# VectorE instead of TensorE turns q and k in an attention with hashed masks and two feed-forward layers

## The chip, the cores and the metric

The kernel runs on one core of one Trainium2 chip. The metric is the time of one execution on the device in microseconds (us); lower is better. The engines of a core work side by side and wait for each other through semaphores only: TensorE (PE, with its weight loads as PEld), VectorE (DVE), ScalarE (ACT), GpSimd (POOL), and SyncE (SP), which here issues nearly all DMA transfers.

## What is computed

Everything is in 32-bit floats. There are 2 batches of 8 heads, 768 positions and 64 columns a head; the output of attention, 1536 x 512, goes through two feed-forward layers.

```python
scale = 1.0 / np.sqrt(D)
q_bits = (np.einsum('bhsd,dk->bhsk', q, proj) > 0).astype(np.int64)
k_bits = (np.einsum('bhsd,dk->bhsk', k, proj) > 0).astype(np.int64)
mask = q_bucket[:, :, :, None] == k_bucket[:, :, None, :]   # buckets: the 6 bits as a number
scores = scale * np.matmul(q, k.transpose(0, 1, 3, 2))
scores = np.where(mask, scores, -1000000000.0)
scores = scores - np.max(scores, axis=-1, keepdims=True)
attn = np.exp(scores)
attn = attn / (np.sum(attn, axis=-1, keepdims=True) + 1e-09)
x = np.matmul(attn, v)
h = np.maximum(np.maximum(x @ w1, x @ w2), x @ w3) @ w_out
g = h @ w_in
out = (g * (1.0 / (1.0 + np.exp(-1.702 * g)))) @ w_out2
```

## The kernel before

The program is written out engine by engine: each engine has its own list of instructions in a fixed order, and every dependence is a wait on a semaphore. An engine never goes past an instruction that waits.

**Heads and tiles.** The 16 heads are taken in 8 pairs. A head's scores are made 128 rows of queries by 768 keys at a time (a score tile); 96 tiles in all. The main loop runs over groups n = 4 to 32 of three tiles each, 3n, 3n+1 and 3n+2, called A, B and C below; four groups make a pair of heads, p = n // 4, st = n % 4. Groups 0 to 3 are written out one by one.

**One group on TensorE.** In order: scores of A (L1522, four matmuls into the PSUM banks psS), three half tiles of probabilities turned with the identity (`turn_probs`, L1530, nine transposes into the ring of three banks psR), scores of B, three more half tiles, scores of C behind them in the next turn of the loop. Between B and C stand twelve matmuls with the values (`times_values`, L1544, into psO) and, depending on st, one of three things: at st 0 and 1 `turn_qk` (L1470), which turns q and k of one head of the next pair, six transposes of 128x128; at st 2 `project` (L1500), which multiplies the turned q and k of both heads with proj; at st 3 nothing. In this text a group's halves are turned as "D": the order on the engine is C, D, A, D, B, values, then the next C.

**The chain of one tile.** VectorE takes the maximum over the scores in PSUM (`row_max`, L1128), ScalarE the exponential with its sum (`exp_tile`, L803), VectorE the guarded sums and their reciprocals (`invert_sums`: lone L1136, lone_sums L1137, guarded L1142, inv L1145), GpSimd the normalization in place (`norm`, L577), TensorE turns it, and ScalarE (L812) or VectorE (L1152) copies the halves out of the ring. Two score banks (psS) mean that the scores of tile i wait for the exponential of tile i − 2. A and B are inverted together, so their lone and lone_sums work on two columns, those of C on one. At even n VectorE also makes x_lo (L1158) between the inversion of A and B and the maximum of C.

**One head's q and k before the scores.** SP loads them (`load_qk`, L436) into w_raw, as rows of positions with q and k side by side: 128 partitions, runs of 64 columns (256 bytes). TensorE turns them into two ring banks. ScalarE copies the banks out (`copy_qk`, L796), with a scale that is −1/8 on the 64 partitions of q and 1 on those of k. GpSimd splits the result into a high part (qk_hi, L560) and the rest (qk_lo, L573), which follow the two norms of its group. SP places the parts into stacks (`place_hi`, `place_lo`, `place_marks`), from which the scores are made one pair later. Buffers for loaded, turned and split heads are there twice, so head m uses those of head m − 2.

GpSimd has more work in some groups: from n = 16 on, at st 2 and 3, three sums of x each (L626), and in the last four groups the first block of weights. Behind attention come the feed-forward layers on TensorE, with their weights split by GpSimd and ScalarE.

Of the kernel before, what the change touches and what calls it, by code (L numbers as in the profile page):

```python
# [5 lines left out]
def lsh_attention_ffn(nc, q, k, v, proj, w1, w2, w3, w_out, w_in2, w_out2, out):  # L6
# [3 lines left out]
    ts = bass.ts  # L10
# [74 lines left out]
    k_r = k.rearrange("b h (p t) d -> (b h) p t d", p=P)  # L85
    v_r = v.rearrange("b h (p t) d -> (b h) p t d", p=P)
    w_up = [w.rearrange("(c p) f -> p c f", p=P) for w in (w1, w2, w3)]
    w_out_r = w_out.rearrange("(c p) d -> p c d", p=P)
# [6 lines left out]
    for n_ in range(GROUPS + 1):  # L95
        p_, st = n_ // 4, n_ % 4
        halves = [("probs", i, j) for i in range(3 * n_ - 3, 3 * n_) for j in range(2)] if n_ > 0 else []
        if n_ == 2:

            ring_order += halves[:2] + [("bits", 1)] + halves[2:]  # L100
            continue
        ring_order += halves[:3]
        if st < 2 and p_ + 1 < PAIRS:
            ring_order += [("turn", 2 * p_ + 2 + st, j) for j in range(2)]
        if st == 2 and p_ + 1 < PAIRS:
            ring_order += [("bits", p_ + 1)]
        ring_order += halves[3:]
# [3 lines left out]
    with ctx:  # L111
# [55 lines left out]
        sum_of_w = sb("sum_of_w", [P, SLOT], F32)  # L167
        qk_raw = [w_raw[:, ts(a, S)].rearrange("p (t s d) -> p t s d", s=2, d=D) for a in range(2)]
        qk_t = [w_raw[:, ts(2 + a, S)] for a in range(2)]
        qk_hi = [w_hi[:, ts(a, S)] for a in range(2)]  # L170
# [88 lines left out]
        dve_stacked = sem("dve_stacked")  # L259
        pool_stacked = sem("pool_stacked")  # L260
        qk_hi_made = sem("qk_hi_made")
        qk_lo_made = sem("qk_lo_made")
# [86 lines left out]


        def hi_stacked(m):
            return hi_placed[m % 2], 64 * (m // 2)
# [75 lines left out]
        def _(sync):  # L428
            def load_qk(m):
                if m >= 4:  # L430
                    sync.wait_ge(*filled(("turn", m - 2, 1)))
                elif m >= 2:
                    sync.wait_ge(first_turned, 2 * (m - 1))
                for which, src in enumerate((q_r, k_r)):
                    if m >= 2 or which == 0:
                        sync.dma_start(qk_raw[m % 2][:, :, which, :], src[m, :, :, :]).then_inc(qk_loaded[m % 2], 16)  # L436
# [28 lines left out]
            def load_block(k):  # L465
                if k == 0:
                    sync.wait_ge(*filled(("turn", HEADS - 1, 1)))
                elif k < 3:
                    sync.wait_ge(*filled(("bits", PAIRS - 1)))
                    sync.wait_ge(qk_lo_made, HEADS - 2)  # L470
                else:
                    sync.wait_ge(w_split, part_use[k - 2, "a11"])
                fp, c = k // 3, k % 3
                sync.dma_start(w_raw[:, ts(k % 3, BLOCK_COLS)].rearrange("p (c f) -> p c f", c=KC),
                               w_up[c][:, :, ts(fp, SLOT)]).then_inc(w_loaded[k % 3], 16)
# [75 lines left out]
        def _(pool):  # L551
# [10 lines left out]
            def make_qk_hi(m):  # L562
                for j in range(2):
                    pool.wait_ge(*emptied(("turn", m, j)))
                if m >= 4:
                    pool.wait_ge(*hi_stacked(m - 2))
                copy(qk_hi[m % 2], qk_t[m % 2]).then_inc(qk_hi_made, 1)
# [220 lines left out]
        def _(act):  # L788
            def copy_qk(m, j):
                act.wait_ge(*filled(("turn", m, j)))  # L790
                if m in (2, 3):
                    act.wait_ge(dve_stacked, m + 1)
                    act.wait_ge(pool_stacked, (2, 6)[m - 2])
                if m >= 4:
                    act.wait_ge(qk_lo_made, m - 3)
                act.activation(half(qk_t[m % 2], j), bank(("turn", m, j))[:, 0:HALF], ACT.Copy,  # L796
                               scale=qk_scale[:, 0:1]).then_inc(bank_emptied(("turn", m, j)), 1)

            def exp_tile(i):
# [81 lines left out]
            for n in range(4, GROUPS + 1):  # L881
# [9 lines left out]
                if st < 2 and p + 1 < PAIRS:  # L891
                    for j in range(2):
                        copy_qk(2 * p + 2 + st, j)
                copy_turned(3 * n - 2, 1)
# [214 lines left out]
        def _(dve):  # L1109
# [11 lines left out]
            def make_first_bits(a):  # L1121
                dve.wait_ge(*filled(("bits", 0, a)))
                dve.tensor_scalar(first_marked[a], bank(("bits", 0, a))[:, 0:HALF], marks[:, 2:3], marks[:, 3:4], ALU.is_gt,
                                  ALU.mult).then_inc(bank_emptied(("bits", 0, a)), 1)

            def row_max(i):
                dve.wait_ge(scores_ready, i + 1)
# [96 lines left out]
            row_max(11)  # L1224
            copy_turned(8, 1)
            for n in range(4, GROUPS + 1):
                p, st = n // 4, n % 4
# [4 lines left out]
                if n < GROUPS:  # L1232
                    row_max(3 * n + 1)
                    invert_sums(3 * n, 2)
                    if st == 2 and p + 1 < PAIRS:
                        make_bits(p + 1)
# [221 lines left out]
        def _(pe):  # L1458
# [33 lines left out]
            def project(p):  # L1492
                for a in range(2):
                    for j in range(2):
                        pe.wait_ge(*emptied(("turn", 2 * p + a, j)))
                o = ring_bank(("bits", p))
# [103 lines left out]
            for n in range(4, GROUPS + 1):  # L1600
# [9 lines left out]
                for c in range(TH * part, TH * part + TH):  # L1610
                    times_values(u, c)
                if st < 2 and p + 1 < PAIRS:
                    turn_qk(2 * p + 2 + st)
                if st == 2 and p + 1 < PAIRS:
# [177 lines left out]
```

## Time and profile before

| | us |
|---|---|
| median of 3 runs | 672.41 (672.07 to 672.5) |
| span of the profiled execution, first to last instruction | 670.8 |
| TensorE busy | 663.7 (99%) |
| VectorE busy | 495.9 (74%) |
| ScalarE busy | 346.6 (52%) |
| GpSimd busy | 474.2 (71%) |
| clock granted to TensorE, mean | 1.000 of full speed |

The span is from the profile; of the profiled execution the profile gives no time other than this span, and the median of the separate runs is 1.6 us above it. Busy times are sums over the instructions of an engine, and those of matmuls are modelled, so that 99% doesn't mean that TensorE couldn't go faster; what it waits for is read from the chain and the timeline. Attention takes the first 230 us or so.

### The profile page before, as it was taken

How to read it: one execution, taken by the hardware profiler on the slowest of the kernel's cores; microseconds unless marked ns; L12 is line 12 of the kernel's file. 1: busy time of each engine (PE TensorE's matmuls, PEld its weight loads, DVE VectorE, ACT ScalarE, POOL GpSimd, SP SyncE). 2: the span in 40 equal slices, each digit the busy share in tenths (PEclk: the TensorE clock that was granted, in tenths of full speed). 3: DMA queues.
4: the chain of work that ended last, by engine and by line, in shares of the span. 5: the costliest groups of instructions: out<-in, count | busy, mean ns of one | idle time of the engine just before them, and what ended most of it. 6: DMA issues, size and time to landing. Idle time of an engine off the chain costs nothing.

```text
span 670.8 us, 11966 instructions
## 1 busy us (share of the span) xinstructions
PE 663.7 (99%) x3892; PEld 576.8 (86%) x3892; DVE 495.9 (74%) x976; ACT 346.6 (52%) x761; POOL 474.2 (71%) x538
## 2 busy tenths in 40 slices
PE   8999999999999999999999999999999999999998
PEld 6776777777777699999999999988898988989896
DVE  6878878788788799869778963678877666555554
ACT  6887777877777630011103453555545554454433
POOL 6774756788876899968870528799987776777710
PEclk9999999999999999999999999999999999999999
DMA  6673836638352111111110201212232124212102
GB/s 159 152 161 102 192 88 155 151 88 187 91 132 75 34 32 32 32 32 33 32 40 25 95 1 33 79 48 80 79 93 64 64 78 143 64 64 65 45 18 94
DMA packets 58492, 54.17 MB, mean 81 GB/s; under 512 B 28640, under 2 KB 47488, under 8 KB 58432
## 3 DMA queue, kind: packets, MB, share of 16 engines
q1 hardware_dynamic: 56784, 53.02, 29.2%
q8 instruction: 32, 0.52, 0.3%
q10 hardware_dynamic: 1648, 0.39, 0.3%
q14 instruction: 28, 0.23, 0.1%
HBM read 32.51 MB, written 3.15 MB: 53 GB/s over the span
## 4 chain that ended last, share of the span: by engine, by line
PE 88%; POOL 6%; issue 2%; ACT 1%; DVE 1%; DMA 1%; DVEq 0%; ACTq 0%; POOLq 0%
PE psO L1544 10%; PE psS L1522 10%; PE psR L1530 9%; PE psR L1628 7%; PE psR L1627 7%; PE psR L1629 7%; PE psS L1627 6%; PE psS L1628 6%; PE psS L1629 6%; PE psS L1730 4%; PE psS L1729 4%; PE psS L1728 4%; POOL w_lo L736 3%; PE psR L1470 1%; POOL w_raw L727 1%
## 5 line engine op out<-in xcount | busy, mean ns | idle before, releaser
L577 POOL TENSOR_SCALAR probs<-probs,lone,inv 128x768 f32<-128x768 f32 x96 | 93.9, 985 | 58.6 <-DVE inv L1145 58.5
L736 POOL TENSOR_TENSOR w_lo<-w_raw,w_hi 128x256 fp32r<-128x256 f32 x96 | 79.2, 838 | 44.6 <-ACT w_hi L982 43.9
L1128 DVE TENSOR_REDUCE neg_max<-psS 128x1 f32<-128x768 f32 x96 | 91.2, 950 | 12.9 <-PE psS L1522 8.7
L803 ACT ACTIVATE probs<-psS,neg_max 128x768 f32<-128x768 f32 x96 | 86.5, 901 | 15.7 <-DVE neg_max L1128 15.6
L560 POOL TENSOR_SCALAR w_hi<-w_raw 128x256 fp32r<-128x256 f32 (+1 forms) x79 | 49.0, 624 | 50.2 <-PE psS L1629 28.9
L812 ACT ACTIVATE probs_t<-psR 128x384 f32<-128x384 f32 x131 | 60.7, 491 | 31.2 <-PE psR L1530 30.7
L1530 PE MATMUL psR<-ident,probs 128*128 128x128 f32 x576 | 74.6, 273 | 0.4 <-POOL probs L577 0.2
L1530 PEld LDWEIGHTS psR<-ident,probs 128*128 128x128 f32 x576 | 66.5, 140 | 5.5 <-POOL probs L577 2.1
L1544 PE MATMUL psO<-probs_t,v_raw 128*64 128x384 f32 x384 | 68.8, 494 | 0.0
L1379 DVE TENSOR_TENSOR v_raw<-psR,early 128x384 f32<-128x384 f32 x64 | 35.3, 552 | 32.4 <-PE psR L1629 32.2
L1384 DVE TENSOR_TENSOR v_raw<-v_raw,bits 128x384 f32<-128x384 f32 x64 | 53.7, 841 | 6.7 <-ACT bits L1005 4.3
L1628 PE MATMUL psR<-x_lo,w_hi 128*128 128x384 f32 x160 | 53.8, 337 | 0.0
L1629 PE MATMUL psR<-x_hi,w_lo 128*128 128x384 f32 x160 | 53.6, 335 | 0.0
L1627 PE MATMUL psR<-x_hi,w_hi 128*128 128x384 f32 x160 | 53.4, 334 | 0.0
L1005 ACT ACTIVATE bits<-v_raw 128x384 f32<-128x384 f32 x64 | 33.5, 524 | 35.9 <-DVE v_raw L1379 35.7
L1544 PEld LDWEIGHTS psO<-probs_t,v_raw 128*64 128x64 f32 x384 | 24.8, 136 | 30.8 <-issue 30.5
L741 POOL TENSOR_TENSOR w_parts<-w_raw,w_parts 128x512 fp32r<-128x512 f32 x32 | 42.1, 1339 | 8.4 <-ACT w_parts L990 8.4
L597 POOL TENSOR_TENSOR w_lo<-w_raw,w_hi 128x256 fp32r<-128x256 f32 x52 | 46.0, 890 | 0.3
L982 ACT ACTIVATE w_hi<-w_raw 128x256 fp32r<-128x256 f32 x87 | 31.9, 406 | 27.0 <-POOL w_raw L727 24.4
L1379 DVE TENSOR_TENSOR early<-psR,early 128x384 f32<-128x384 f32 x48 | 26.5, 552 | 25.8 <-PE psR L1629 25.6
L1302 DVE TENSOR_TENSOR probs_t<-probs_t,v_raw 128x384 f32<-128x384 f32 x48 | 35.0, 748 | 0.0
L1152 DVE COPY probs_t<-psR 128x384 f32<-128x384 f32 x61 | 33.6, 551 | 0.7
(275 smaller groups left out, 1881.5 us busy)
## 6 DMA issues: line engine op xcount, KB each, us to landing
w_raw<-in_moe_w_in SPq DMA_DIRECT2D x16, 512.0 KB, 3.4
w_raw<-in_moe_w_out SPq DMA_DIRECT2D x32, 256.0 KB, 2.7
w_raw<-in_moe_w SPq DMA_DIRECT2D x9, 512.0 KB, 3.8
h_lo<-w_hi SPq DMA_DIRECT2D x22, 192.0 KB, 3.3
h_hi<-w_hi SPq DMA_DIRECT2D x18, 192.0 KB, 3.4
w_raw<-in_q SPq DMA_DIRECT2D x16, 192.0 KB, 3.6
v_raw<-in_v SPq DMA_DIRECT2D x16, 192.0 KB, 2.5
stacks<-w_hi SPq DMA_DIRECT2D x16, 192.0 KB, 3.3
```

The costliest lines, as they stand in the source:

```text
L577: pool.tensor_scalar(probs[i % PROBS][:, :], probs[i % PROBS][:, :], lone[:, i % 6:i % 6 + 1], inv[:, i % 6:i % 6 + 1], ALU.add, ALU.mult) ...
L736: pool.tensor_tensor(in2_slot(w_lo, n, which), in2_raw(n, PARTS2[which]), f32(in2_slot(w_hi, n, which)), ALU.subtract).then_inc(in2_split, 1)
L803: act.activation(probs[i % PROBS][:, :].rearrange("p (a b) -> p a b", a=2), psS[i % 2][:, :, 0:HALF], ACT.Exp, bias=neg_max[:, i % 6:i % 6 ...
L812: act.activation(probs_t[u % 2][:, s // TH, ts(j, TH), ts(s % TH, P)], bank(("probs", i, j))[:, 0:HALF].rearrange("p (c q) -> p c q", c=TH ...
L1128: dve.tensor_reduce(neg_max[:, i % 6:i % 6 + 1], psS[i % 2][:, :, 0:HALF], AX.XY, ALU.min).then_inc(max_ready, 1)
L1379: dve.tensor_tensor(o, psU[(7 * n + product) % 2], other, ALU.add).then_inc(mix_added, 1)
L1522: mm = pe.matmul(psS[i % 2][:, j, 0:HALF], stack(n, qs)[0:rows, ts(t, P)], half(stack(n, ks)[0:rows, :], j), start=which == 0, stop=which ...
L1530: mm = pe.transpose(o[:, ts(c, P)], probs[i % PROBS][:, ts(j * TH + c, P)], ident[:, :])
L1544: mm = pe.matmul(psO[a * D:(a + 1) * D, 0:HALF], v_raw[p % 2][a][:, c, :], probs_t[u % 2][:, a, c, :], start=c == 0, stop=c == NT - 1)
L1627: pe.matmul(o, wh, xh, start=c == 0, stop=False)
L1628: pe.matmul(o, wh, xl, start=False, stop=False)
L1629: mm = pe.matmul(o, wl, xh, start=False, stop=c == len(terms) - 1)
```

## The change

For heads 4 to 15, `turn_qk` and `copy_qk` go. Instead:

- SP loads each head in four transfers (q and k, the lower and the upper 32 columns) into `qk_swap`, the same memory seen otherwise: 32 partitions each, one for a position out of 32, with 24 runs of 32 columns (128 bytes).
- VectorE turns all 128 partitions by 768 columns in one instruction (`swap_qk`), which works on blocks of 32x32. The layout of the load makes the result the same as before, with q not yet scaled. It stands in VectorE's list before the main loop (head 4), at st 0 behind the maximum of B (head 2p+3) and at st 3 at the same place (head 2p+4).
- ScalarE multiplies the 64 partitions of q by −1/8 in place (`scale_q`), where it copied the banks out.
- GpSimd's split and `project` wait for `scale_q`, the next load of the buffer for `swap_qk`. The ring no longer holds the turned heads.

```diff
-                if m >= 4:
+                if m >= 6:
+                    sync.wait_ge(qk_swapped, m - 5)
+                elif m >= 4:
                     sync.wait_ge(*filled(("turn", m - 2, 1)))
...
+                for which, src in enumerate((q_s, k_s) if m >= 4 else ()):
+                    for e in range(2):
+                        sync.dma_start(qk_swap[m % 2][32 * (2 * which + e):32 * (2 * which + e) + 32, :, :].rearrange(
+                            "p (t g) c -> p t g c", t=NT), src[m, e, :, :, :, :]).then_inc(qk_loaded[m % 2], 16)
...
+            def scale_q(m):
+                act.wait_ge(qk_swapped, m - 3)
+                act.activation(qk_t[m % 2][0:D, :], qk_t[m % 2][0:D, :], ACT.Copy, scale=NEG_SCALE).then_inc(q_scaled, 1)
...
                 if st < 2 and p + 1 < PAIRS:
-                    for j in range(2):
-                        copy_qk(2 * p + 2 + st, j)
+                    scale_q(2 * p + 2 + st)
...
+            def swap_qk(m):
+                dve.wait_ge(qk_loaded[m % 2], 64 * (m // 2))
+                dve.wait_ge(*filled(("bits", m // 2 - 1)))
+                dve.wait_ge(qk_lo_made, m - 3)
+                dve.transpose(qk_t[m % 2].rearrange("p (n r) -> p n r", r=32), qk_swap[m % 2]).then_inc(qk_swapped, 1)
...
             copy_turned(8, 1)
+            swap_qk(4)
             for n in range(4, GROUPS + 1):
...
                     row_max(3 * n + 1)
+                    if st == 0 and p + 1 < PAIRS:
+                        swap_qk(2 * p + 3)
+                    if st == 3 and p + 2 < PAIRS:
+                        swap_qk(2 * p + 4)
                     invert_sums(3 * n, 2)
...
-                if st < 2 and p + 1 < PAIRS:
-                    turn_qk(2 * p + 2 + st)
                 if st == 2 and p + 1 < PAIRS:
                     project(p + 1)
```

On TensorE at n = 5, before the change: the last product with the values, the transposes of one head, and the scores and halves behind them.

```order
L1544 MATMUL psO<-probs_t,v_raw_1 64x384
L1470 MATMUL psR<-ident,w_raw 128x128 x6
L1522 MATMUL psS<-stacks 128x384 x4
L1530 MATMUL psR<-ident,probs 128x128 x9
L1522 MATMUL psS<-h_lo 128x384 x4
L1530 MATMUL psR<-ident,probs 128x128 x9
```

The same place on TensorE in the changed kernel.

```order
L1570 MATMUL psO<-probs_t,v_raw_1 64x384
L1548 MATMUL psS<-stacks 128x384 x4
L1556 MATMUL psR<-ident,probs 128x128 x9
L1548 MATMUL psS<-h_lo 128x384 x4
L1556 MATMUL psR<-ident,probs 128x128 x9
```

The scores of C now stand directly behind the products with the values; nothing else moved on this engine.

On VectorE at n = 8, before: from the maximum of B to the maximum of C and the copy behind it.

```order
L1128 TENSOR_REDUCE neg_max<-psS 128x1
L1136 TENSOR_SCALAR lone<-neg_max 128x2
L1137 TENSOR_SCALAR lone_sums<-neg_max 128x2
L1142 TENSOR_SCALAR guarded<-sums,lone_sums 128x1 x2
L1145 RECIPROCAL inv<-guarded 128x2
L1158 TENSOR_TENSOR x_lo<-psO,x_hi 128x384
L1128 TENSOR_REDUCE neg_max<-psS 128x1
L1152 COPY probs_t<-psR 128x3x128
```

The same place on VectorE in the changed kernel.

```order
L1149 TENSOR_REDUCE neg_max<-psS 128x1
L1145 STREAM_TRANSPOSE w_raw<-w_raw 128x768
L1157 TENSOR_SCALAR lone<-neg_max 128x2
L1158 TENSOR_SCALAR lone_sums<-neg_max 128x2
L1163 TENSOR_SCALAR guarded<-sums,lone_sums 128x1 x2
L1166 RECIPROCAL inv<-guarded 128x2
L1179 TENSOR_TENSOR x_lo<-psO,x_hi 128x384
L1149 TENSOR_REDUCE neg_max<-psS 128x1
```

The transpose has come between the maximum of B and the inversion of A and B; everything behind it keeps its order. At st 3 it is the same without x_lo.

## Rows read from the trace of the kernel before

**Rows 1.** The page: busy us (share of the span), for each engine

```profile
PE 663.7 (99%) x3892; PEld 576.8 (86%) x3892; DVE 495.9 (74%) x976; ACT 346.6 (52%) x761; POOL 474.2 (71%) x538
```

**Rows 2.** Chain of waits, 100 to 121 us: start, length, what

```profile
100.09 0.81 PE psR L1470 x6
...
107.03 0.78 PE psR L1500 x8
...
114.18 0.90 PE psS L1522 x4
...
116.06 0.70 PE psS L1522 x4
116.76 0.98 PE psR L1530 x9
117.74 0.69 PE psS L1522 x4
...
120.53 0.81 PE psR L1470 x6
```

**Rows 3.** Timeline, 115 to 125 us: start, length, instruction [idle before it]

```profile
115.06 1.95 POOL L577 TENSOR_SCALAR probs<-probs,lone,inv 128x768 f32<-128x768 f32 x2 [1.47 <-DVE inv L1145]
115.11 0.96 DVE L1128 TENSOR_REDUCE neg_max<-psS 128x1 f32<-128x768 f32 x1
...
116.20 0.90 ACT L803 ACTIVATE probs<-psS,neg_max 128x768 f32<-128x768 f32 x1
116.42 1.08 PEld L1530 LDWEIGHTS psR<-ident,probs 128*128 128x128 f32 x9
...
117.47 0.65 PEld L1522 LDWEIGHTS psS<-h_hi 128*128 128x128 f32 x4
...
118.78 0.94 DVE L1128 TENSOR_REDUCE neg_max<-psS 128x1 f32<-128x768 f32 x1
...
119.82 0.17 DVE L1136 TENSOR_SCALAR lone<-neg_max 128x2 f32<-128x2 f32 x1
...
120.77 0.33 DVE L1142 TENSOR_SCALAR guarded<-sums,lone_sums 128x1 f32<-128x1 f32 x2 [0.72 <-ACT probs L803]
...
121.22 0.54 DVE L1158 TENSOR_TENSOR x_lo<-psO,x_hi 128x384 fp32r<-128x384 f32 x1
...
121.41 1.95 POOL L577 TENSOR_SCALAR probs<-probs,lone,inv 128x768 f32<-128x768 f32 x2 [1.47 <-DVE inv L1145]
...
124.24 1.83 POOL L573 TENSOR_TENSOR w_lo<-w_raw,w_hi 128x768 fp32r<-128x768 f32 x1
```

**Rows 4.** Groups of instructions: operation, shapes, count | busy us, mean ns

```profile
L1128 DVE TENSOR_REDUCE neg_max<-psS 128x1 f32<-128x768 f32 x96 | 91.2, 950 | 12.9 <-PE psS L1522 8.7
...
L1250 DVE TENSOR_TENSOR h_lo<-probs,h_lo 128x768 fp32r<-128x768 f32 x3 | 4.5, 1487 | 0.0
...
L828 ACT ACTIVATE h_hi<-w_raw 64x768 fp32r<-64x768 f32 x2 | 1.7, 845 | 0.5 <-DVE w_raw L1186 0.5
...
L1189 DVE CAST h_hi<-w_raw 64x768 fp32r<-64x768 f32 x1 | 0.6, 558 | 0.1
```

**Rows 5.** Timeline at 30 and at 174 us, VectorE and GpSimd

```profile
30.29 1.81 POOL L573 TENSOR_TENSOR w_lo<-w_raw,w_hi 128x768 fp32r<-128x768 f32 x1
30.38 1.75 DVE L1136 TENSOR_SCALAR lone<-neg_max 128x2 f32<-128x2 f32 x1
...
173.55 0.94 DVE L1128 TENSOR_REDUCE neg_max<-psS 128x1 f32<-128x768 f32 x1
...
174.90 0.98 POOL L577 TENSOR_SCALAR probs<-probs,lone,inv 128x768 f32<-128x768 f32 x1
```

**Rows 6.** Timeline of VectorE, the maximum of tile 13

```profile
36.61 0.94 DVE L1128 TENSOR_REDUCE neg_max<-psS 128x1 f32<-128x768 f32 x1
```

**Rows 7.** Loads of q: from issue to landing

```profile
L436 SPq DMA_DIRECT2D w_raw<-in_q x16: 540/599/873, 0.7 to 155.7; - x16
...
DMA to landing us min/median/max: 3.0/3.6/4.7
```

More of the change, by code:

```diff
@@ L86, in lsh_attention_ffn @@
     v_r = v.rearrange("b h (p t) d -> (b h) p t d", p=P)
+    q_s, k_s = (x.rearrange("b h (g r t) (e c) -> (b h) e r t g c", g=P // 32, r=32, c=32) for x in (q, k))
     w_up = [w.rearrange("(c p) f -> p c f", p=P) for w in (w1, w2, w3)]
@@ L102, in lsh_attention_ffn @@
         ring_order += halves[:3]
-        if st < 2 and p_ + 1 < PAIRS:
+        if st < 2 and p_ == 0:
             ring_order += [("turn", 2 * p_ + 2 + st, j) for j in range(2)]
@@ L168, in lsh_attention_ffn @@
         qk_raw = [w_raw[:, ts(a, S)].rearrange("p (t s d) -> p t s d", s=2, d=D) for a in range(2)]
+        qk_swap = [w_raw[:, ts(a, S)].rearrange("p (n r) -> p n r", r=32) for a in range(2)]
         qk_t = [w_raw[:, ts(2 + a, S)] for a in range(2)]
@@ L260, in lsh_attention_ffn @@
         pool_stacked = sem("pool_stacked")
+        qk_swapped = sem("qk_swapped")
+        q_scaled = sem("q_scaled")
         qk_hi_made = sem("qk_hi_made")
@@ L348, in bank, with qk_ready @@
             return psR[ring_use[key] % RING]
+        def qk_ready(m):
+            return [(q_scaled, m - 3)] if m >= 4 else [emptied(("turn", m, j)) for j in range(2)]
         def hi_stacked(m):
@@ L433, in load_qk @@
                     sync.wait_ge(first_turned, 2 * (m - 1))
+                for which, src in enumerate((q_s, k_s) if m >= 4 else ()):
+                    for e in range(2):
+                        sync.dma_start(qk_swap[m % 2][32 * (2 * which + e):32 * (2 * which + e) + 32, :, :].rearrange(
+                            "p (t g) c -> p t g c", t=NT), src[m, e, :, :, :, :]).then_inc(qk_loaded[m % 2], 16)
                 for which, src in enumerate((q_r, k_r)):
-                    if m >= 2 or which == 0:
+                    if 2 <= m < 4 or m < 2 and which == 0:
                         sync.dma_start(qk_raw[m % 2][:, :, which, :], src[m, :, :, :]).then_inc(qk_loaded[m % 2], 16)
@@ L466, in load_block @@
                 if k == 0:
-                    sync.wait_ge(*filled(("turn", HEADS - 1, 1)))
+                    sync.wait_ge(qk_swapped, HEADS - 4)
                 elif k < 3:
@@ L562, in make_qk_hi @@
             def make_qk_hi(m):
-                for j in range(2):
-                    pool.wait_ge(*emptied(("turn", m, j)))
+                for ready in qk_ready(m):
+                    pool.wait_ge(*ready)
                 if m >= 4:
@@ L793, in copy_qk @@
                     act.wait_ge(pool_stacked, (2, 6)[m - 2])
-                if m >= 4:
-                    act.wait_ge(qk_lo_made, m - 3)
                 act.activation(half(qk_t[m % 2], j), bank(("turn", m, j))[:, 0:HALF], ACT.Copy,
                                scale=qk_scale[:, 0:1]).then_inc(bank_emptied(("turn", m, j)), 1)
+            def scale_q(m):
+                act.wait_ge(qk_swapped, m - 3)
+                act.activation(qk_t[m % 2][0:D, :], qk_t[m % 2][0:D, :], ACT.Copy, scale=NEG_SCALE).then_inc(q_scaled, 1)
             def exp_tile(i):
@@ L891, in _ @@
                 if st < 2 and p + 1 < PAIRS:
-                    for j in range(2):
-                        copy_qk(2 * p + 2 + st, j)
+                    scale_q(2 * p + 2 + st)
                 copy_turned(3 * n - 2, 1)
@@ L1493, in project @@
                 for a in range(2):
-                    for j in range(2):
-                        pe.wait_ge(*emptied(("turn", 2 * p + a, j)))
+                    for ready in qk_ready(2 * p + a):
+                        pe.wait_ge(*ready)
                 o = ring_bank(("bits", p))
```

## The prediction

> **What bounds the kernel now.** First the page: TensorE is busy 99% of the span, VectorE 74% [rows 1]. A busy share proves little here, since ends of matmuls are modelled, so the chain of waits comes next. From 100 to 121 us it holds nothing but TensorE, back to back; of the repeating pieces [rows 2] show one of each kind. A group n takes three score tiles, A, B and C (3n, 3n+1, 3n+2), and in the chain the stretch from the end of one group's twelve products with the values to the end of the next one's has one of three lengths. With turn_qk in it: 107.03 − 100.09 = 6.94 us. With project: 114.18 − 107.03 = 7.15. With neither: 120.53 − 114.18 = 6.35. That third kind is the one to study: it is what every turning group becomes, and it is already measured, with the other engines keeping up.
>
> Then the timeline around n = 15 and 16, to see how narrowly they keep up [rows 3]. VectorE starts the maximum of tile B at 118.78 (call it s). ScalarE's exponential follows, then VectorE's guarded sums at 120.77 = s+1.99, GpSimd's normalization of two tiles at 121.41 = s+2.63 for 1.95 us. One group earlier, those two normalizations end at 117.01, and TensorE's weight load for the third half of the next nine transposes comes about 0.72 us after 116.42, at 117.14: 0.13 us of margin. The other loop is maximum, exponential, next scores: the maximum of C at 115.11 gives probabilities at about 115.11 + 1.09 + 0.90 + 0.05 = 117.15 (its exponential starts at 116.20, 1.09 later, and takes 0.90; 0.05 is my allowance for the signal), and the weight load of B at 117.47 needs them: 0.3 us of margin. So the bound is TensorE's time, with VectorE and GpSimd 0.1 to 0.3 us behind it.
>
> **What is removed.** Heads 4 to 15 lose turn_qk, six transposes each, in twelve groups (n = 4p and 4p+1, p = 1 to 6). Priced by the transposes alone it would be 0.81 us [rows 2]. But scores that start right behind the products with values take 0.90 us in the chain instead of 0.69 (as at 114.18 [rows 2]), so the group saves 6.94 − 6.35 = 0.59, say 0.60. Twelve groups: **−7.2 us**, if nothing else ends later. ScalarE loses two copies a head and gets one multiplication over 64x768; such an activation took 0.845 us [rows 4]. It stands where ScalarE waits for TensorE's halves today, and GpSimd has its result before it is through with the norms, so I cost it at nothing; without that cover it would be 0.85 us in front of a copy that frees a ring bank.
>
> **What is added: the transpose on VectorE.** No row has this operation. Nearest rows for 768 columns [rows 4]: a one-source cast of 64x768 took 0.558 us, the reduction over 768 columns 0.950, a two-source subtraction of 128x768 beside a working GpSimd 1.49. I take 1.0 us (T): it is one-source work over as many columns as the reduction, and I add a little for the reordering. Ends for the range: 0.56 and 1.49.
>
> The Trainium skill speaks against the trade. Its page "VectorE: DVE Perf Modes", section "The three transpose paths" and the rules behind it, gives 311 ns for a 128x128 block in bf16 on VectorE and says to use TensorE where PSUM will do as destination. Six such blocks would be an estimate of 1.87 us a head if no fixed part is shared, and by that the change would lose (the rival below reaches the same size from rows). Its page "Vector Engine (DVE) Microarchitecture Reference", section 3.8, has the transpose sustain one element a cycle, which is nearer to my 1.0. No run here shows either yet.
>
> Where it stands matters more than its length. It follows the maximum of B and precedes the guarded sums, where VectorE today waits 0.72 us for the exponential [rows 3]. The maximum hands over at s+0.87 (its length less the 0.09 us by which records overlap), the transpose holds VectorE until s+1.78, the two small operations lone and lone_sums follow (0.17 us each, mostly overlapped: I allow 0.33 to what comes after them), and the guarded sums come at s+2.11 instead of s+1.99. **The transpose is almost wholly hidden: 0.12 us late.** What is late then:
> - n = 4p+3 (five groups): the norms end 0.12 later, against 0.13 of margin. About 0.05 us each.
> - n = 4p, p = 2 to 6 (five groups): x_lo (0.54 us) follows too, and C now starts at once. C would end at 120.53 + 0.89 = 121.42, VectorE comes to it at s+2.11+0.45+0.50 = 121.84 (0.45 is from the guarded sums to x_lo, 0.50 is x_lo less its overlap), and the next B's probabilities are there at 123.88; its weight load is due at 121.42 + 0.98 + 0.70 + 0.98 − 0.27 = 123.81. About 0.1 us each. Together 0.75 us.
> - n = 4: two transposes in one group's time, the first before the maximum of tile 12. The maximum of tile 13, at 36.61 today [rows 6], starts about 0.68 late, the second transpose adds 0.12, x_lo and C's maximum follow, all near 1.0 us late against some 0.4 of margin: 0.6 us.
>
> **The other cost: GpSimd.** The rows show that a small two-column operation of VectorE can be held for the whole of a GpSimd instruction: lone over 128x2 took 1.75 us from 30.38, ending as GpSimd's subtraction from 30.29 (1.81 us) ended [rows 5]; otherwise it takes 0.17 (119.82 [rows 3]). (By the Trainium skill, "SBUF — State Buffer", section "Who interferes with whom", the two engines share a port pair as an exclusive lock, and one-source operations outside the two-port modes don't take it. The trace agrees for the two-column operations; for the transpose nothing here shows it yet.) GpSimd's last piece of a head, qk_lo, ends 4.66 us after the two norms began (121.41 to 124.24 + 1.83 [rows 3]), that is at s+7.29. With a period of 6.94 it is over 0.35 us into the next period and lone, due at 1.04, passes between it and the end of the norm behind it. With 6.35 it is over at 0.94, and the next norm (0.98 us) starts at about the moment lone comes. If it wins, lone ends near 2.05 and the guarded sums come 0.3 us late, 0.25 of it beyond the margin. Six groups (n = 4p+1), at even odds with 0.3 each: 0.9 us; the six project groups behind them, which have project as cover: 0.3 us. At n = 20 and 24 GpSimd's sums of x of the group before push that norm to s+1.35 (174.90 beside a maximum at 173.55 [rows 5]); lone, moved to s+1.78 by the transpose, is held until s+2.33, and the guarded sums come 0.6 late: 0.5 us beyond margin, twice, 1.0 us.
>
> **Loads.** Each head's q and k come as 4 transfers of 32 partitions with runs of 128 bytes instead of 2 with 256, twice the packets. Now such a load lands 3.6 us after issue in the median, 4.7 at most [rows 7]. Between the transpose that frees the buffer and the one that needs it again lie three or four groups, 19 us or more. Even four times 4.7 us fits. Nothing; uncovered, every microsecond past 19 holds the in-order VectorE and so TensorE. SP issues 24 more transfers (0.6 us each) with waits of several us between heads: nothing.
>
> **Sum.** −7.2 + 0.75 + 0.6 + 0.9 + 0.3 + 1.0 = −3.65 us. The span of 670.8 becomes 667.15; the median of the runs, 672.41, lies 1.6 above the span, so **668.8 us**. Behind attention TensorE stays at full load on weights, and I expect the gain to carry to the end.
>
> **Rivals.**
> 1. The stalls are absorbed (orders fall well, the lock favours VectorE): only n = 4 loses. For it: the free groups run at 6.35 today without one wait, and margins are taken from modelled ends. −6.6 us, 665.8. Chance 0.24.
> 2. **VectorE becomes the bound, slower.** The place is the transpose before the guarded sums, at n = 4p and 4p+3; price T. Each 0.1 us over 1.0 goes through the norms to TensorE eleven times. At half a reduction's rate, T is some 1.75 to 1.9: 11 × 0.75 = 8.25 us more, net +4.6, 677. At 1.49, +5.4, net +1.75, 674.2. It decides at T = 1.0 + 3.65/11 = 1.33 us. Against it: both one-source rows of [rows 4] stay under 1.0 us for 768 columns. Chance 0.13.
> 3. The loads come too late, because packets of 128 bytes to 32 partitions are far slower. They must take over 19 us where 4.7 is the most now. Each us above costs ten or more: say +3, 675. Chance 0.04.
> 4. A wash: the lock costs 0.3 to 0.5 us in all twelve groups behind qk_lo and the stalls add up to 6 or 7 us. 671.1 to 673.7. Chance 0.11.
> 5. My forecast, 667 to 671: chance 0.48.
>
> Faster by over 0.2% (1.3 us, about what a measurement tells from no change): 0.24 + 0.48 = 0.72. Same 0.11, slower 0.17. The range goes from the full saving, 665.2, to T = 1.49, 674.2; it leaves out what of rivals 2 and 3 lies above and a full hiding below, some 0.15.
>
> **What would show it.** Transposes of about 1.0 us, eleven of them between a maximum and lone; free, former turning groups at 6.35 to 6.5 us in the chain, n = 4 near 6.95, n = 20 and 24 near 6.95; guarded sums at s+2.1. Wrong if a transpose takes over 1.3 us, if VectorE waits on a load, if lone over 128x2 is long in most groups, or if TensorE waits for GpSimd's norms more than a few tenths a group.

## The result and the profile after

| | before | after |
|---|---|---|
| median of 4 runs, us | 672.24 (672.04 to 672.5) | 666.71 (666.22 to 666.98) |
| ratio after / before | | 0.9917, 95% interval 0.9903 to 0.9931 |
| span of the profiled execution, us | 670.8 | 664.4 |

The change makes the kernel 5.53 us faster (672.24 − 666.71). The forecast was 668.8, which foresaw 3.6; the range held the time. The profiled execution took 666.22 us, 1.8 more than its span; the spans of the other three runs were 664.9, 664.9 and 665.2. The unedited changed kernel measured again beside experiments 10 to 12 took 666.81 us (0.9917, 0.9904 to 0.9931).

First the page of after, the line of busy times, against [rows 1]:

```profile
PE 657.3 (99%) x3820; PEld 569.4 (86%) x3820; DVE 505.1 (76%) x988; ACT 343.6 (52%) x749; POOL 474.2 (71%) x538
```

TensorE has 72 instructions and 6.4 us fewer, VectorE 12 more and 9.2 us more. As before, the share proves little, so the chain of waits of after comes next (start, length, what), at the groups n = 13 and 14:

```profile
95.38 2.09 PE psO L1570 x12
97.46 0.89 PE psS L1548 x4
...
101.72 2.09 PE psO L1570 x12
103.81 0.78 PE psR L1526 x8
```

A group that turned q and k has lost its piece of six transposes, and the products with the values begin 101.72 − 95.38 = 6.34 us apart, where such groups took 6.94 [rows 2]. Read for all groups, the distances from one group's products with the values to the next one's are (in us, named by the group n whose turn of VectorE or TensorE lies in them):

| groups | before | after |
|---|---|---|
| n = 5, 9, 13, 17 and 8, 12, 16 | 6.94 to 6.95 | 6.35 to 6.37 |
| n = 4 | 6.95 | 6.88 |
| n = 20, 24 | 6.94 to 6.95 | 6.80, 6.80 |
| n = 21, 25 | 6.95 | 6.36, 6.36 |
| st = 2 (project) | 7.14 to 7.15 | 7.14 to 7.15 |
| st = 3 | 6.34 to 6.35 | 6.34 to 6.35 |

Nine groups gave the whole 0.59; n = 4 kept 0.07, and n = 20 and 24 kept 0.14 each. Nothing else moved. That is 9 × 0.59 + 0.07 + 2 × 0.14 = 5.7 us of attention. Read directly, the products with the values behind n = 27, past the last changed group, start at 194.72 where they started at 200.60: 5.9 us, of which 0.2 is there before the first changed group. Nothing of it is given back later. So the difference of the two spans (6.4) has two parts that the change didn't make: those 0.2 us of the start (the second group's products begin at 29.6 before and 29.4 after, and anywhere from 29.4 to 30.1 in the profiles of this study), and 0.4 us at 562.6, where TensorE in the profile of before stands still behind VectorE, back to a load of weights (`w_raw<-in_moe_w_in` in its chain of waits); the profile of after has no such wait there.

The groups of instructions of after, different shapes apart (line, engine, operation, shapes, count | busy us, mean ns | idle before):

```profile
L1145 DVE STREAM_TRANSPOSE w_raw<-w_raw 128x768 f32<-128x768 f32 x12 | 11.6, 969 | 0.0
L1157 DVE TENSOR_SCALAR lone<-neg_max 128x2 f32<-128x2 f32 x31 | 10.1, 325 | 1.8
L813 ACT ACTIVATE w_raw<-w_raw 64x768 f32<-64x768 f32 x12 | 10.0, 834 | 0.0
```

The new transpose takes 0.969 us, and VectorE never stood idle before it, so no load was late. ScalarE's multiplication takes 0.834 us and nothing waits for it. The loads of q and k of heads 4 to 15 in the changed kernel (L446), from issue to landing:

```profile
DMA to landing us min/median/max: 2.9/3.9/4.8
```

A transfer now carries 768 runs of 128 bytes where it carried 768 of 256, and lands in 3.9 us instead of 3.6 [rows 7]; a head has four of them instead of two.

**A group where it is hidden, and one where it isn't.** The timeline of after at n = 19 (135 to 140 us) and n = 20 (141 to 147 us):

```profile
135.39 0.94 DVE L1149 TENSOR_REDUCE neg_max<-psS 128x1 f32<-128x768 f32 x1
136.24 0.97 DVE L1145 STREAM_TRANSPOSE w_raw<-w_raw 128x768 f32<-128x768 f32 x1
136.36 0.90 ACT L819 ACTIVATE probs<-psS,neg_max 128x768 f32<-128x768 f32 x1 [0.54 <-DVE neg_max L1149]
137.13 0.12 DVE L1157 TENSOR_SCALAR lone<-neg_max 128x2 f32<-128x2 f32 x1
137.44 0.33 DVE L1163 TENSOR_SCALAR guarded<-sums,lone_sums 128x1 f32<-128x1 f32 x2
138.07 1.94 POOL L591 TENSOR_SCALAR probs<-probs,lone,inv 128x768 f32<-128x768 f32 x2 [1.14 <-DVE inv L1166]
...
141.74 0.94 DVE L1149 TENSOR_REDUCE neg_max<-psS 128x1 f32<-128x768 f32 x1
142.59 0.97 DVE L1145 STREAM_TRANSPOSE w_raw<-w_raw 128x768 f32<-128x768 f32 x1
143.13 0.98 POOL L591 TENSOR_SCALAR probs<-probs,lone,inv 128x768 f32<-128x768 f32 x1
143.49 0.65 DVE L1157 TENSOR_SCALAR lone<-neg_max 128x2 f32<-128x2 f32 x1
144.30 0.34 DVE L1163 TENSOR_SCALAR guarded<-sums,lone_sums 128x1 f32<-128x1 f32 x2
144.94 1.94 POOL L591 TENSOR_SCALAR probs<-probs,lone,inv 128x768 f32<-128x768 f32 x2 [0.83 <-DVE inv L1166]
...
145.97 0.64 PEld L1556 LDWEIGHTS psR<-ident,probs 128*128 128x128 f32 x6 [0.23 <-POOL probs L591]
...
146.93 0.31 PEld L1556 LDWEIGHTS psR<-ident,probs 128*128 128x128 f32 x3 [0.33 <-POOL probs L591]
```

At n = 19 the transpose lies beside ScalarE's exponential, and the guarded sums start at 137.44 = s+2.05 (s is the start of the maximum of B), 0.06 later than before [rows 3]. At n = 20 GpSimd's norm, late through the sums of x, starts at 143.13, before lone comes; lone over two columns ends with it at 144.14 instead of about 143.6, the guarded sums stand at s+2.56, and TensorE's weight loads wait 0.23 and 0.33 us for the norms. At n = 24 lone is held for 0.65 us too, at 170.14.

The timeline of after at n = 4, where two transposes fall into one group's time:

```profile
34.21 0.97 DVE L1145 STREAM_TRANSPOSE w_raw<-w_raw 128x768 f32<-128x768 f32 x1
...
37.04 0.94 DVE L1149 TENSOR_REDUCE neg_max<-psS 128x1 f32<-128x768 f32 x1
...
37.90 0.97 DVE L1145 STREAM_TRANSPOSE w_raw<-w_raw 128x768 f32<-128x768 f32 x1
...
40.77 0.64 PEld L1556 LDWEIGHTS psR<-ident,probs 128*128 128x128 f32 x6 [0.33 <-POOL probs L591]
...
41.73 0.31 PEld L1556 LDWEIGHTS psR<-ident,probs 128*128 128x128 f32 x3 [0.32 <-POOL probs L591]
```

The maximum of tile 13 starts at 37.04, 0.43 later than [rows 6]. The products with the values ahead of this group start at 36.03 here and at 36.21 before, so against its own group it is 0.61 late. TensorE waits 0.33 and 0.32 us for the norms of A and B.

### The profile page after: what moved, and what is told of

Same layout as the page of the kernel before. It is cut to its first block, busy times and chain, and to the rows that moved or that the text cites. A ratio compares the mean times of both kernels' runs of the same rounds, so it can differ in the third digit from the quotient of the medians.

```text
span 664.4 us, 11816 instructions
## 1 busy us (share of the span) xinstructions
PE 657.3 (99%) x3820; PEld 569.4 (86%) x3820; DVE 505.1 (76%) x988; ACT 343.6 (52%) x749; POOL 474.2 (71%) x538
## 4 chain that ended last, share of the span: by engine, by line
PE 90%; POOL 4%; issue 3%; DVE 2%; ACT 1%; DVEq 0%; POOLq 0%
PE psR L1652 8%; PE psR L1653 8%; PE psR L1651 8%; PE psS L1548 8%; PE psO L1570 8%; PE psR L1556 7%; PE psS L1651 6%; PE psS L1652 6%; PE psS L1653 6%; PE psS L1754 4%; PE psS L1753 4%; PE psS L1752 4%; POOL probs L591 2%; PE psR L1753 1%; PE psO L1754 1%
## 5 line engine op out<-in xcount | busy, mean ns | idle before, releaser
L1410 DVE TENSOR_TENSOR v_raw<-v_raw,bits 128x384 f32<-128x384 f32 x64 | 51.5, 806 | 5.7 <-ACT bits L1020 2.9
```

## Experiments

Each kernel is the changed kernel with one edit, timed against the kernel before in five rounds; medians in us. "Interval" is the distance between the products with the values, as in the table above. The medians of the kernel before, beside experiments 1 to 4, 5 to 8 and 9 to 12, are 672.31, 671.99 and 672.27, so a difference of two medians across these groups is good to some 0.3 us only; the intervals don't depend on that.

**1. small_swap: how much do the transposes cost in all?** One block of 32 columns is turned instead of 24; the other columns of q and k of heads 4 to 15 are left as they are, so this kernel leaves out part of the computation.

```diff
-dve.transpose(qk_t[m % 2].rearrange("p (n r) -> p n r", r=32), qk_swap[m % 2]).then_inc(qk_swapped, 1)
+dve.transpose(qk_t[m % 2][:, 0:32], qk_swap[m % 2][:, 0, :]).then_inc(qk_swapped, 1)
```

> Takes the cost away: VectorE turns only 32 of the 768 columns of each head (the rest of q and k keeps old data, so this leaves out part of the computation); all waits stay. Theory A (the transpose fits the wait for the exponential, but makes n = 4, 20 and 24 late by 0.4 to 0.5 us each): those three groups go back to 6.35 us and the time falls by 1.3 to 1.5 us, to about 665.3. Rival B (the transpose costs nothing anywhere, and the three late groups are due to GpSimd alone): 666.7, no change.

665.09 (664.75 to 665.49), ratio 0.9895 (0.988 to 0.9911). From the groups of this kernel:

```profile
L1145 DVE STREAM_TRANSPOSE w_raw<-w_raw 128x32 f32<-128x32 f32 x12 | 2.4, 202 | 0.0
```

All twelve intervals are 6.34 to 6.35, those of n = 4, 20 and 24 too. So the removal alone is worth 672.31 − 665.09 = 7.2 us, and the length of the transposes costs 666.71 − 665.09 = 1.6.

**2 and 3. longer_swap and double_swap: when is the cover used up?** Ahead of each transpose stands another one, of 256 columns in longer_swap and of all 768 in double_swap, which the real one waits for.

```diff
 dve.wait_ge(qk_lo_made, m - 3)
+dve.transpose(qk_t[m % 2][:, 0:2 * P].rearrange("p (n r) -> p n r", r=32), qk_swap[m % 2][:, 0:2 * P // 32, :]).then_inc(spare_made, 1)
+dve.wait_ge(spare_made, m - 3)
```

> Each head's transpose is preceded by one of 256 more columns, which it waits for: some 0.5 us more in the same place. Theory A (about 0.1 us of margin behind the transpose, then every tenth goes to TensorE, eleven times in the main loop): 11 x 0.4 = +4.4 us, 671.1; the turning point against before, an added 0.5 us, is just reached. Rival B (VectorE has a quarter of its time free, so a longer transpose is absorbed): at most +1 us.

> Each head is turned twice, the second after the first: about 1.05 us more in the same place. Theory A: 11 x 0.95 = +10.5 us, 677, slower than before the change. Rival B: at most +2 us, since the whole adds 12 us of VectorE work to 505 of 664.

longer_swap: 670.44 (670.25 to 671.06), ratio 0.9976 (0.9967 to 0.9986). double_swap: 677.77 (676.01 to 678.1), ratio 1.0077 (1.0064 to 1.0089). The groups of longer_swap:

```profile
L1148 DVE STREAM_TRANSPOSE w_raw<-w_raw 128x768 f32<-128x768 f32 x12 | 11.7, 978 | 0.4
L1146 DVE STREAM_TRANSPOSE w_raw<-w_raw 128x256 f32<-128x256 f32 x12 | 5.2, 435 | 0.0
```

VectorE is held 1.45 us at each place instead of 0.97 (from 118.78 to 120.23 at n = 16), and the kernel loses 3.7 us of the gain. The intervals say where: those of n = 4p+3 grow from 6.35 to 6.75 (6.81 at n = 19), those of n = 8, 12 and 16 by 0.15 and of n = 20 and 24 by 0.07 and 0.09, that of n = 4 to 7.86. The timeline of longer_swap behind n = 15 shows the route:

```profile
114.61 1.96 POOL L592 TENSOR_SCALAR probs<-probs,lone,inv 128x768 f32<-128x768 f32 x2 [2.00 <-DVE inv L1169]
...
115.66 0.64 PEld L1559 LDWEIGHTS psR<-ident,probs 128*128 128x128 f32 x6 [0.20 <-POOL probs L592]
...
116.62 0.31 PEld L1559 LDWEIGHTS psR<-ident,probs 128*128 128x128 f32 x3 [0.32 <-POOL probs L592]
```

The late guarded sums make the norms late, and TensorE's transposes wait for each of the two. In double_swap VectorE is held 1.98 us (117.27 to 119.25) and the intervals reach 7.28 at n = 4p+3 (7.33 at n = 19), 7.02 at n = 4p, 6.72 at n = 5 and 9.84 at n = 4. The first 0.48 us costs 3.7 in all, the next 0.53 costs 7.3.

Not all of those 7.3 us are VectorE's delay. At n = 4 TensorE stands still for 1.75 us, and its granted clock falls. The timeline of double_swap:

```profile
43.44 1.86 PE L1559 MATMUL psR<-ident,probs 128*128 128x128 f32 x9 [1.75 <-POOL probs L592]
```

From 44 to 47 us, with TensorE at work again, its granted clock is 0.50 of full speed, the lower of its two levels, and these nine transposes take 1.86 us where others take 1.15. Four of the five runs have a mean clock of 0.997 and took 677.24 to 678.1; the one at 1.000 took 676.01. At full clock, then, the second step costs about 5.6, still more than the first.

**4. behind_inv: is it the place that hides it?** The inversion of A and B goes ahead of the transpose.

```diff
 row_max(3 * n + 1)
+invert_sums(3 * n, 2)
 if st == 0 and p + 1 < PAIRS:
     swap_qk(2 * p + 3)
 if st == 3 and p + 2 < PAIRS:
     swap_qk(2 * p + 4)
-invert_sums(3 * n, 2)
```

> The same transpose, but behind the inversion of A and B instead of before it. Theory A (only the hole in which VectorE waits for the exponential hides it): the norms come on time, but the maximum of C starts 0.6 us late at st 3 and 1.1 us late at st 0 against 0.3 of margin: 5 x 0.3 + 6 x 0.9 = +6.9 us, about 673.5. Rival B (any place in the list would do, because VectorE is busy only 76%): within 0.5 us of 666.7.

672.25 (671.67 to 672.49), ratio 0.9997 (0.9988 to 1.0005): the whole gain is gone by the order of two steps on VectorE. The intervals are 6.68 at n = 4p+3, 7.11 at n = 4p, 7.76 at n = 4. The chain of waits of behind_inv at n = 16, which holds only TensorE there in the changed kernel:

```profile
121.02 0.35 DVE guarded L1163 x2
...
121.50 0.30 DVE w_raw L1145
...
...
122.92 0.56 DVE neg_max L1149
...
123.71 0.55 DVE probs_t L1173
...
124.39 0.52 PE psR L1556 x3
```

VectorE waits for the exponential as before, starts the transpose when it should already be at x_lo and the maximum of C, and the copy that frees a ring bank comes 0.33 us late for TensorE. The time was expected at about 673.5, so the place costs 1.2 us less than foreseen.

**5. early_swap4: is n = 4 late because of its second transpose?** The transpose of head 4 moves from in front of the loop to a place ahead of the inversion of tiles 9 and 10, beside an exponential like the others.

```diff
 copy_turned(6, 0)
+swap_qk(4)
 invert_sums(9, 2)
...
 copy_turned(8, 1)
-swap_qk(4)
```

> Head 4 is turned earlier, before the inversion of tiles 9 and 10, where VectorE's lone is held for 1.7 us by GpSimd in any case. Theory A: the group n = 4 then has one transpose like n = 8, its interval falls from 6.87 to about 6.35 us, and the time falls by 0.5 us, to 666.2. Rival C (the transpose, SBUF to SBUF, is held by GpSimd's instruction like lone): the transpose there takes over 1.5 us or stands behind GpSimd's, and the gain is below 0.2 us.

666.19 (665.71 to 666.53), ratio 0.9913 (0.99 to 0.9927). The interval of n = 4 goes from 6.88 to 6.35, 0.53 us. The difference of the medians (666.71 − 666.19 = 0.52) agrees better than it can be trusted to. The new place also shows what the prediction couldn't. The timeline of early_swap4 at 31 us:

```profile
30.80 1.84 POOL L587 TENSOR_TENSOR w_lo<-w_raw,w_hi 128x768 fp32r<-128x768 f32 x1
30.92 0.97 DVE L1145 STREAM_TRANSPOSE w_raw<-w_raw 128x768 f32<-128x768 f32 x1
31.81 0.85 DVE L1157 TENSOR_SCALAR lone<-neg_max 128x2 f32<-128x2 f32 x1
```

Beside GpSimd's two-source subtraction the transpose takes its usual 0.97 us; the two-column lone right behind it is held until that subtraction ends at 32.64. (The Trainium skill, "SBUF — State Buffer", section "Who interferes with whom", has one-source operations outside the two-port modes go beside GpSimd without the lock. The trace fits that for the transpose, 0.97 us beside the subtraction; which mode it runs in no run here shows.)

**6 and 7. lone_first_two and lone_first_all: is n = 20 and 24 the held lone?** lone and lone_sums go ahead of the transpose, at n = 20 and 24, or at every transpose of the loop; the guarded sums stay behind it.

```diff
-def invert_sums(i, count):
+def invert_sums(i, count, between=None):
...
                   ALU.mult).then_inc(lone_found, 1)
+if between is not None:
+    swap_qk(between)
 dve.wait_ge(probs_ready, i + count)
```

> At n = 20 and 24 alone, lone and lone_sums stand before the transpose, so that they are over before GpSimd's delayed norm begins. Theory A: lone over two columns falls from 0.65 us to under 0.25 in both groups, their intervals from 6.8 to about 6.4 us, and the time falls by 0.8 us, to 665.9. Rival D (GpSimd is late there because of its three sums, however VectorE is ordered): no change, 666.7.

> The same order, lone and lone_sums before the transpose, in all eleven groups of the main loop. At n = 20 and 24 as in the run with these two alone, -0.8 us; in the other nine the guarded sums come about 0.15 us later, which is about the margin that the run with the longer transpose left (11 x 0.5 minus 3.7 is 1.8, 0.16 each). Theory A: 665.9 to 666.3. Rival D: 666.7 or more.

lone_first_two: 665.79 (665.71 to 666.37), ratio 0.991 (0.9896 to 0.9923); both intervals fall from 6.80 to 6.50, and 0.15 over the free groups is left. lone_first_all: 667.46 (667.28 to 667.66), ratio 0.9933 (0.992 to 0.9947), a miss: it is 0.75 us slower than the changed kernel, where a gain was expected. Its intervals are 6.64 and 6.67 at n = 19 and 23, 6.68 at n = 8, and 6.59 and 6.58 at n = 20 and 24, which together are 0.5 us more than in the changed kernel. The timeline of lone_first_all at n = 19:

```profile
137.04 0.98 POOL L591 TENSOR_SCALAR probs<-probs,lone,inv 128x768 f32<-128x768 f32 x1
137.48 0.56 DVE L1157 TENSOR_SCALAR lone<-neg_max 128x2 f32<-128x2 f32 x1
138.01 0.97 DVE L1145 STREAM_TRANSPOSE w_raw<-w_raw 128x768 f32<-128x768 f32 x1
138.91 0.29 DVE L1165 TENSOR_SCALAR guarded<-sums,lone_sums 128x1 f32<-128x1 f32 x2
```

The group before is one in which GpSimd makes sums of x, so its norm for C is late here too. In the changed kernel the transpose filled that time, and lone came when the norm was over (137.13, 0.12 us, above). Moved ahead, lone is held, and holds the transpose with it. The expectation had looked only at groups where lone behind the transpose is held. At n = 8 the transpose starts 0.29 us after lone_sums, at 65.45, with nothing shown that it waits for; that one stays open.

**8. both: do the two remedies add up?** Edits 5 and 6 together.

> Head 4 turned early and lone first at n = 20 and 24. Theory A: the two effects are in different groups and add: -1.3 us, 665.4, what the small transpose reached (665.1) less nothing else. Rival: the saved time is given back behind attention, and the time stays above 666.

665.85 (665.61 to 665.89), ratio 0.9908 (0.9895 to 0.9922). The intervals are those of each edit (6.35 at n = 4; 6.49 and 6.49 at n = 20 and 24), so the groups add up to −1.15 us. The median gained 0.86 against the changed kernel and was expected at 665.4; the rest is within the 0.3 us named above.

**9. after_again**: the changed kernel unedited, beside experiments 10 to 12.

> The changed kernel once more, unedited, beside the others of this call. Every theory: 666.7, within 0.3 us.

666.81 (666.23 to 667.04), the same within 0.1 us.

**10. double_loads: how far are the loads from mattering?** Each head is loaded a second time into the same place; SP waits until the first loads have landed, and VectorE waits for the second.

```diff
+if m >= 4:
+    sync.wait_ge(qk_loaded[m % 2], 128 * (m // 2) - 128)
+for which, src in enumerate((q_s, k_s) if m >= 4 else ()):
+    for e in range(2):
+        sync.dma_start(... the same load again ...).then_inc(qk_loaded[m % 2], 16)
...
-dve.wait_ge(qk_loaded[m % 2], 64 * (m // 2))
+dve.wait_ge(qk_loaded[m % 2], 128 * (m // 2) - 64)
```

> From head 4 on, each head is loaded twice, the second time after the first has landed, and VectorE waits for the second: twice the packets and twice the time to landing. Theory A (the loads have three to four groups of time, so their 128-byte runs cost nothing): no change, 666.7 within 0.5 us. Rival E (the new loads are near their limit, and part of what the change gives is lost to them): VectorE waits for loads, and the time rises by 3 us or more.

710.15 (709.45 to 711.27), ratio 1.0565 (1.0551 to 1.058): 43.3 us slower than the changed kernel beside it, by far the largest miss of this study. The rival's sign came true and its mechanism didn't: in the groups of this kernel the transposes have no idle time before them, so VectorE never waits for a load. The intervals show a loss of 5.7 to 9.3 us once in each pair, where the scores of the next pair begin (14.65 us at n = 7). From the waits of TensorE's weight loads and of SP in double_loads (engine, line <- releaser: us, times, longest):

```profile
PEld psS L1554 <- DMA h_lo<-w_hi: 17.3, 3, 7.4
...
SPq L452 <- DMA w_raw<-in_k: 28.7, 12, 2.8
```

and its timeline at 76 us, behind n = 7:

```profile
76.55 0.50 PEld L1554 LDWEIGHTS psS<-h_hi 76*128 76x128 f32 x2 [6.81 <-DMA h_hi<-w_hi]
```

TensorE waits for the transfers that place the parts and marks of a head into the stacks (L470 to L482), 32.7 us in all (17.3 above and 15.4 more behind h_hi). These transfers stand behind the loads in SP's order. (While TensorE stands still from 70 us on, its granted clock falls to 0.50 of full speed, and it stays low over the first 3 us of work, to 79 us; the mean of the run is 0.973.) SP's timeline says how tight that order is. First the changed kernel, then double_loads:

```profile
61.98 1.41 SPq L446 DMA_DIRECT2D w_raw<-in_q  x2
63.43 1.36 SPq L446 DMA_DIRECT2D w_raw<-in_k  x2
68.72 2.78 SPq L464 DMA_DIRECT2D h_lo<-w_hi  x4
```

```profile
58.73 1.77 SPq L446 DMA_DIRECT2D w_raw<-in_q  x2
60.55 2.42 SPq L446 DMA_DIRECT2D w_raw<-in_k  x2
65.04 1.28 SPq L452 DMA_DIRECT2D w_raw<-in_q  x2
66.36 1.36 SPq L452 DMA_DIRECT2D w_raw<-in_k  x2
67.83 0.60 SPq L470 DMA_DIRECT2D h_hi<-w_hi  x1
```

In the changed kernel SP is done with a head's loads at 64.79 and next starts at 68.72: 3.93 us, nearly all of its free time in this pair (4.2 to 5.3 in the next three). The experiment makes a head's loads last 8.99 us instead of 2.81 (58.73 to 67.72) and those of the other head 7.83 instead of 2.93 (79.99 to 87.82): 11.1 us more a pair. Less the 3.93 free, that is 7.2 us a pair, and the mean loss is 43.3 / 6 = 7.2. The equality is partly luck, since the single losses and SP's free time differ from pair to pair. But SP's timeline in double_loads has no gap left other than the waits for the first loads, so SP had become the bound; what TensorE loses at the lower clock runs beside SP's work and needn't add to it. How it divides between the four further issues and the wait for the landing was not tried; the change itself has no such wait.

**11. one_column: is it the two columns that are held?** lone and lone_sums are made one column at a time everywhere.

```diff
-dve.tensor_scalar(lone[:, cols], neg_max[:, cols], MASKED / 2, LONE, ALU.is_ge, ALU.mult).then_inc(lone_found, 1)
...
+split = True
+for to, value in ((lone, LONE), (lone_sums, S * LONE)):
+    for part in ([slice(c, c + 1) for c in range(i % 6, i % 6 + count)] if split else [cols]):
+        dve.tensor_scalar(to[:, part], neg_max[:, part], MASKED / 2, value, ALU.is_ge,
+                          ALU.mult).then_inc(lone_found, 1 if split else count)
...
-dve.wait_ge(lone_found, 2 * inverted(i))
+dve.wait_ge(lone_found, 2 * (i + count))
```

> lone and lone_sums of A and B are made one column at a time, in all groups. Theory A (GpSimd holds VectorE's small operation only where it spans two columns): no lone is ever longer than 0.2 us, n = 20 and 24 give back 0.4 us each, and the 0.12 us that two more instructions add stays within the 0.16 us of margin elsewhere: 665.9 to 666.3. Rival F (any small operation of VectorE is held there): 666.7 or more, with long rows of lone left.

665.89 (665.65 to 666.36), ratio 0.9906 (0.9893 to 0.992). The timeline of one_column at n = 20, which answers to 143.13 and 143.49 of the changed kernel:

```profile
144.18 0.98 POOL L591 TENSOR_SCALAR probs<-probs,lone,inv 128x768 f32<-128x768 f32 x1
144.42 0.17 DVE L1160 TENSOR_SCALAR lone<-neg_max 128x1 f32<-128x1 f32 x2
```

Two one-column instructions pass within 0.17 us beside the norm that held the two-column one for 0.65. The intervals of n = 20 and 24 are 6.35; the 96 lones take 110 to 155 ns each. The price is two short instructions more in every group: n = 4 rises from 6.88 to 7.00.

**12. best: the two small losses removed.** Edit 5, and edit 11 at n = 20 and 24 alone.

> Head 4 turned early, and lone and lone_sums one column at a time at n = 20 and 24 alone. Theory A: -0.5 and -0.8 us, 665.3 to 665.5, all groups of the main loop at 6.35 us (7.15 with project) as with the small transpose. Rival: no better than 666.2, because what is saved comes back as a wait elsewhere.

665.45 (664.93 to 665.49), ratio 0.9897 (0.9884 to 0.9911). All twelve intervals are 6.34 to 6.39. It is 1.3 us faster than the changed kernel and 6.8 faster than the kernel before, and 0.4 us short of the 665.09 of small_swap, whose transposes cost next to nothing. No other kernel here that does the whole work is faster.

## Why the prediction was right, and the terms that were too large

**The removal, −7.2 us.** Shown: small_swap is 7.2 us below before, and nine groups of the changed kernel lost 0.59 each. The third kind of group in the profile of before, measured without turn_qk, was the right thing to read it from; pricing the six transposes would have given 0.81 a group.

**T = 1.0 us.** Measured 0.969. The lengths 0.202, 0.435 and 0.969 us for 32, 256 and 768 columns lie on one line: 1.04 ns a column and 0.17 us fixed. That settles the two statements that the prediction weighed. The Trainium skill's 311 ns for one 128x128 block ("VectorE: DVE Perf Modes", "The three transpose paths") agrees with this line, though it is for bf16: the line gives 0.30 for 128 columns. More than half of that is the fixed part, which one instruction over six blocks pays once, and that is why six times the figure, 1.87, came out nearly twice as long as the 0.969; six instructions in a row no run here has. The Trainium skill's one element a cycle ("Vector Engine (DVE) Microarchitecture Reference", section 3.8) fits a slope that is constant from 32 to 768 columns; how long a cycle is no run here shows. The Trainium skill's rule to use TensorE where PSUM will do ("VectorE: DVE Perf Modes", "Rules for kernel authors") doesn't ask which engine has time to spare. Here TensorE was the bound and VectorE had a wait to fill, and 666.71 against 672.24 decides against the rule.

**Hidden behind the exponential.** Shown by behind_inv: at another place the same instructions cost 5.5 us more. The guarded sums stand at s+2.05 (n = 4 and 19), where s+2.11 was worked out.

**Where the sum was too large.** −3.65 was foreseen, −5.53 measured. The time lies inside the range and just outside the band of 667 to 671 that the forecast gave a chance of 0.48. Three terms that the prediction gave as losses did not come: "about 0.05 us each" at n = 4p+3 and "about 0.1 us each" at n = 4p (0.75 together), the lock "at even odds with 0.3 each" at n = 4p+1 (0.9), and the project groups behind them (0.3). That is 1.95 us, and the difference is 1.9. So the gain and the three small losses were rightly foreseen, and these three further losses weren't there. For the first two the step that failed is the margin, taken to a tenth from modelled ends of matmuls: longer_swap needed 0.48 us more of VectorE to lengthen the groups n = 4p+3 by 0.40 and n = 8, 12 and 16 by 0.15, so in the changed kernel these still had about 0.1 and 0.3 us left, where the prediction had them past the end by 0.05 and 0.1. double_swap gives the same two margins (1.01 us more of VectorE, 0.93 and 0.67 longer). For the lock, lone and the norm do meet at n = 4p+1, and lone takes 0.17 to 0.21 us each time. At n = 5, 21 and 25 its record starts 0.01 to 0.02 us ahead of the norm's (44.34 and 44.35), at n = 9, 13 and 17 it starts 0.06 to 0.08 behind (70.57 and 70.51), and GpSimd's records are rough at that scale. So the rows don't say who comes first, and that lone passes at all six places is seen, not explained.

**The small losses.** n = 4: foreseen 0.6, measured 0.53, shown by early_swap4. The size was right and the route only in part: the prediction had the delay go on through x_lo and the maximum of C, and the timeline of after has TensorE wait for the norms of A and B. n = 20 and 24: foreseen 0.5 each, measured 0.45 each, shown by one_column, which takes away exactly this. Three project groups have a held lone too (0.84 to 0.86 us at n = 6, 22 and 26) and lose nothing, since project stands behind them as cover.

**Loads: nothing.** Right for the landing. For SP the step "waits of several us between heads: nothing" held, with less room than it says: the kernel before leaves SP free for about 10 us in a pair, the changed kernel for 4 to 5, and double_loads shows what comes when that is used up.

**The rivals.** What happened is nearest to rival 1, and its 665.8 lies 0.9 below the result. Rival 2, VectorE as the bound, is real but begins further out than the 1.33 us given: between 1.45 us, which still gains 1.9, and 1.98, which loses 5.5; a straight line between them crosses at about 1.6. Its slope of eleven times the excess seems to hold over the whole stretch (11.06 us for 1.01), but by luck: the first half is cushioned by the margins, and some 1.8 us of the second are the lower clock.

## What to carry to other kernels

An operation that is moved off the bounding engine costs what its place makes of it: find the engine's wait for another one, put the work into it, and count what comes later from there, in a group that does without the work already. A small operation that is put behind or ahead of such work moves too, and where it then meets a GpSimd instruction it can cost more than the moved work does (0.45 us at each of n = 20 and 24, where the transposes at most other places cost nothing): look at every group of a kind, not at one. And the free time of an in-order DMA queue is a margin like that of an engine, to be read off its timeline before issues or waits are added to it.

## What the runs showed of the hardware

- The same small operation is held by GpSimd or not according to its columns: lone over 128x2 took up to 1.73 us in the changed kernel while GpSimd worked (at 30.17; 0.65 at n = 20 and 24), over 128x1 in one_column 0.11 to 0.16 in all 96 cases. Only one and two columns were tried.
- The transpose of 128x768 in 32 bits took 967 to 970 ns twelve times in the changed kernel, whatever GpSimd did beside it.
- A transfer of 768 runs of 128 bytes landed 3.9 us after its issue in the median, one of 768 runs of 256 bytes 3.6.
- A delay of VectorE isn't additive: the first half microsecond (longer_swap) lengthened n = 8, 12 and 16 by 0.15 us, the second (double_swap) by 0.52.
- TensorE's granted clock fell to 0.50 of full speed after it had stood still for 1.75 us at n = 4 of double_swap (0.50 from 44 to 47 us), and in each long wait of double_loads; in the changed kernel the mean is 0.999.
